# Fused gated scan, token mixing and two MLPs on one core: the opening's loads and instruction lists reordered, four value buffers, token mixing with its rows in two parts

## What is computed

```python
mag = np.sqrt(a_re * a_re + a_im * a_im)
scale = np.minimum(mag, 0.999) / (mag + 1e-06)
for t in range(S):                       # complex gated linear recurrence, one state per head
    S_re, S_im = ar * S_re - ai * S_im + kv, ar * S_im + ai * S_re   # kv = outer(k_t, v_t)
    y[:, :, t] = einsum('bhd,bhde->bhe', q[:, :, t], S_re)
x = y.transpose(0, 2, 1, 3).reshape(B, S, H * D)
h = np.maximum(x.transpose(0, 2, 1) @ w_tok1, 0.0) @ w_tok2          # token mixing, inner width 256
u = x + h.transpose(0, 2, 1)
x = u + np.maximum(u @ w_ch1, 0.0) @ w_ch2                           # first MLP, 384 -> 1536 -> 384
xn = (x - mean(x)) / sqrt(var(x) + 1e-6) * g_ln
out = x + np.maximum(xn @ w2_ch1, 0.0) @ w2_ch2                      # second MLP
```

## Time and profile before

| | |
|---|---|
| runs | 885.18, 884.48, 885.17 us |
| profiled execution | 885.37 us, of which the span of its instructions is 883.3 us |
| PE busy | 827.5 us (94%), mean granted clock 0.982 |
| DVE, ACT, GpSimd busy | 472.0 us (53%), 421.9 us (48%), 25.3 us (3%) |
| DMA | 71.15 MB, mean 81 GB/s |
| PE's first product | 24.67 us into the span |
| first `up` product of the MLP | 119.43 us into the span |

### The profile page before, as it was taken

The page is one execution under the profiler, slowest core; times in us unless marked ns, Lnnn a source line. Parts: engine busy times, 40 slices in busy tenths (PEclk is TensorE's granted clock), DMA queues, the critical chain, the costliest instruction groups (busy, mean ns, idle before and its releaser), DMA issues.

```text
span 883.3 us, 16477 instructions
## 1 busy us (share of the span) xinstructions
PE 827.5 (94%) x6890; PEld 805.5 (91%) x6890; DVE 472.0 (53%) x811; ACT 421.9 (48%) x760; POOL 25.3 (3%) x39
## 2 busy tenths in 40 slices
PE   0677899999999999999999999999999999999998
PEld 0566799999999999999999999999999999999997
DVE  7786787787586787577743644263133213312121
ACT  8866977877476777377743422222112111211111
POOL 1001001000000010001000000000000000000000
PEclk9869999999999999999999999999999999999999
DMA  9949845454434464135533500000020002000000
GB/s 374 232 66 239 200 77 123 82 109 89 101 81 83 89 134 113 45 88 105 98 64 113 182 1 1 1 1 28 1 81 1 28 1 81 27 1 27 1 27 27
DMA packets 46556, 71.15 MB, mean 81 GB/s; under 512 B 5008, under 2 KB 38032, under 8 KB 45968
## 3 DMA queue, kind: packets, MB, share of 16 engines
q1 hardware_dynamic: 46480, 70.09, 33.1%
HBM read 42.86 MB, written 8.26 MB: 58 GB/s over the span
## 4 chain that ended last, share of the span: by engine, by line
PE 49%; DMA 1%; DVE 1%; SPq 0%; issue 0%; ACT 0%; DVEq 0%
PE bank L367 16%; PE bank L369 16%; PE bank L368 16%; PE bank L1685 1%; DMA rows<-hats 1%; PE bank L1594 0%; SPq L520 0%; PE bank L1612 0%; PE bank L1616 0%; PE bank L1582 0%; DVE turned_x L1334 0%; DVE x_u L1273 0%; DVE hats L1188 0%; DVE qk_t L1175 0%; PE bank L1629 0%
## 5 line engine op out<-in xcount | busy, mean ns | idle before, releaser
L803 ACT ACTIVATE hidden<-bank 128x384 fp32r<-128x384 f32 x192 | 94.1, 490 | 347.3 <-PE bank L369 346.9
L1258 DVE SCALAR_TENSOR_TENSOR hidden<-bank,hidden 128x384 fp32r<-128x384 f32 x192 | 106.1, 553 | 256.6 <-ACT hidden L803 256.4
L369 PE MATMUL bank<-ch,hidden 128*128 128x384 f32 x576 | 192.9, 335 | 0.0
L367 PE MATMUL bank<-ch,hidden 128*128 128x384 f32 x576 | 192.7, 335 | 0.0
L368 PE MATMUL bank<-ch,hidden 128*128 128x384 f32 x576 | 192.4, 334 | 0.0
L367 PEld LDWEIGHTS bank<-ch,hidden 128*128 128x128 f32 x576 | 108.1, 188 | 0.9 <-DVE hidden L1258 0.5
L368 PEld LDWEIGHTS bank<-ch,hidden 128*128 128x128 f32 x576 | 108.1, 188 | 0.0
L369 PEld LDWEIGHTS bank<-ch,hidden 128*128 128x128 f32 x576 | 108.1, 188 | 0.0
L367 PE MATMUL bank<-turned_x,ch 128*128 128x384 f32 x288 | 102.6, 356 | 1.9 <-DVE turned_x L1334 1.9
L369 PE MATMUL bank<-turned_x,ch 128*128 128x384 f32 x288 | 96.9, 336 | 0.0
L368 PE MATMUL bank<-turned_x,ch 128*128 128x384 f32 x288 | 96.8, 336 | 0.0
(11 more groups left out here) (176 smaller groups left out, 1432.3 us busy)
## 6 DMA issues: line engine op xcount, KB each, us to landing
rows<-hats SPq DMA_DIRECT2D x120, 128.5 KB, 4.7
a_t<-in_a_rows_dram SPq DMA_DIRECT2D x18, 384.0 KB, 5.3
qk_t<-in_qk_rows_dram SPq DMA_DIRECT2D x18, 384.0 KB, 5.3
v_t<-in_v_cols_dram SPq DMA_DIRECT2D x24, 192.0 KB, 5.2
plain_ch<-in_moe_w_ch_dram SPq DMA_DIRECT2D x6, 768.0 KB, 7.2
out_dram<-x_u SPq DMA_DIRECT2D x24, 192.0 KB, 2.0
x_kept_dram<-x_u SPq DMA_DIRECT2D x18, 192.0 KB, 3.3
x_u<-x_kept_dram SPq DMA_DIRECT2D x18, 192.0 KB, 3.2
```

Source lines behind the costliest of these rows:

```text
L367: nc.tensor.matmul(ps, lhs_h, rhs_h, start=first, stop=False, skip_group_check=True)
L369: return nc.tensor.matmul(ps, lhs_l, rhs_h, start=False, stop=final, skip_group_check=True)
L803: nc.scalar.activation(hid_h[:, m % NHID, :], hid_ps[m % 2][:, 0:HALF], ACT.Relu).then_inc(hidden_rounded, 1)
L1258: nc.vector.scalar_tensor_tensor(out=hid_l[:, m % NHID, :], in0=hid_ps[m % 2][:, 0:HALF], scalar=0.0, in1=hid_h[:, m % NHID, :].bitcast(F3 ...
```

## The change

The loads on the queue stand in another order, and rows are laid in halves with other DMAs allowed between; `v_t` has four buffers in the first batch (`v_slot`), so that a load waits for tile n-4; the lists of ACT and DVE for the opening are reordered, with the logarithm and exponential steps of unit 1 and some of unit 2 ahead of the cosines of unit 0 and fewer table switches; 34 filler products instead of 26 at the start, and 4 new ones in the first token mixing. In token mixing the first products run rt by rt, the banks are laid anew, and the transposes stand between products. The slow path's buffers move to other places.

```diff
-        v_t = alloc(a_ctx, "v_t", [P, 2, C])
+        v_t = alloc(a_ctx, "v_t", [P, 4, C])
...
+        def v_slot(n):
+            return n % 4 if n < NT else n % 2
...
         def mix_ps(b):
-            return [banks[n] for n in ((0, 1, 7, 2, 3, 4) if b else (5, 6, 7, 0, 1, 4))]
-
-        turn_ps = [banks[n] for n in (5, 6, 7, 2, 3, 4)]
+            return [banks[n] for n in ((0, 1, 7, 2, 3, 4) if b else (0, 1, 4, 5, 6, 7))]
+
+        def turn_ps(b):
+            return [banks[n] for n in ((5, 6, 7, 2, 3, 4) if b else (2, 3, 4, 5, 6, 7))]
...
             def load_v(n):
...
-                if n > 1:
-                    sp.wait_ge(outputs_ready, 2 * (n - 1))
-                    sp.wait_ge(chunk_states, links(n - 1))
-                sp.dma_start(v_t[:, n % 2, :], v_cols[n]).then_inc(loaded_v[n % 2], 16)
+                before = max((i for i in range(n) if v_slot(i) == v_slot(n)), default=None)
+                if before is not None:
+                    sp.wait_ge(outputs_ready, 2 * (before + 1))
+                    sp.wait_ge(chunk_states, links(before + 1))
+                sp.dma_start(v_t[:, v_slot(n), :], v_cols[n]).then_inc(loaded_v[v_slot(n)], 16)
...
             load_a(0)
             load_a(1)
             load_qk(0)
+            load_look(0)
+            load_v(0)
+            load_a(2)
+            load_look(1)
+            load_a(3)
             load_qk(1)
-            for i in range(LOOKS):
-                load_look(i)
+            load_v(1)
             load_piece(0)
-            load_a(2)
-            load_v(0)
-            load_v(1)
+            load_look(2)
+            load_v(2)
+            load_look(3)
             load_piece(1)
-            load_a(3)
-            lay_rows(0)
-            lay_rows(1)
+            lay_rows(0, 0)
+            lay_rows(0, 1)
+            lay_rows(1, 0)
+            load_v(3)
+            lay_rows(1, 1)
+            lay_rows(2, 0)
+            lay_rows(2, 1)
+            load_a(4)
             load_qk(2)
...
@@ decay @@
+                if n == 2:
+                    act.wait_ge(looks_done, 2)
@@ rest, ACT @@
                 keep_x(0, slow)
                 round_x(0)
-                keep_khat(1, 1)
+                keep_khat(1, 0)
                 use_logs()
+                log_abs2(2)
                 inverse_mag(2)
...
@@ opening, ACT @@
             use_turns()
             angle(0)
+            angle(1)
             use_logs()
+            log_abs2(1)
+            inverse_mag(1)
+            log_re(2)
+            square_eps(1)
+            log_eps(1)
             grow_q(0)
             shrink_k(0)
+            square(2)
+            inverse_re(2)
+            grow_q(1)
+            shrink_k(1)
             use_turns()
-            angle(1)
-            decay(0)
             abs_of_turns(0)
             cosine(0)
             sine(0)
-            use_logs()
-            log_abs2(1)
-            square(2)
+            decay(0)
+            abs_of_turns(1)
+            round_piece(act, 0)
             decay(1)
...
@@ opening, DVE @@
             carry_turns(0)
+            half_turn(1)
+            offset_turns(1)
+            sum_turns(1)
+            log_step(1)
+            log_scan(1)
+            round_turns(1)
             grown_qk(0)
+            ratio0(2)
+            wrap(1)
+            carry_turns(1)
+            inverse_check(2)
             hat(0, 0)
             hat(0, 1)
             hat(1, 0)
-            half_turn(1)
             hat(1, 1)
-            offset_turns(1)
+            grown_qk(1)
+            rest_piece(dve, 0)
             least(0)
-            sum_turns(1)
+            hat(2, 0)
             abs2(2)
...
@@ mix_tokens, PE @@
                 pe.wait_ge(khat_kept, 2 * NT * (b + 1))
+                for rt in range(RT):
+                    for j in mix_order(b) if b else (NT - 1,):
+                        mix_down(b, rt, j)
                 pe.wait_ge(pieces_split, SPLIT_AT[1])
-                for j in mix_order(b) if b else (NT - 1,):
-                    for rt in range(RT):
-                        mix_down(b, rt, j)
                 if b:
                     pe.wait_ge(x2_kept, b * NT)
...
+                    pe.wait_ge(tok_hidden_split, b * RT + 1)
                     for j in range(NT):
+                        mix_up(b, 0, j)
+                    pe.wait_ge(tok_hidden_split, b * RT + 2)
+                    for j in range(NT - 1):
+                        mix_up(b, 1, j)
+                    for i in range(CT):
+                        turn_u(b, i)
+                    mix_up(b, 1, NT - 1)
+                    for i in range(CT, 2 * CT):
+                        turn_u(b, i)
+                else:
+                    for i in range(4):
+                        keep_busy()
+                    pe.wait_ge(tok_hidden_split, RT)
+                    for j in range(NT):
+                        for rt in range(RT):
+                            mix_up(b, rt, j)
+                        if j == CT:
+                            for i in range(CT):
+                                turn_u(b, i)
...
             pe.wait_ge(hats_done, 1)
-            for i in range(26):
+            for i in range(34):
                 keep_busy()
...
                         up(m)
+                        if m == 0:
+                            for i in range(CT, 2 * CT):
+                                turn_u(0, i)
+                            pe.wait_ge(u_split, 2 * CT - 1)
```

More of the change, by code:

```diff
@@ L865, in rest @@
                 log_eps(2)
-                decay(3)
+                keep_khat(1, 1)
                 keep_x(1, slow)
                 log_re(3)
+                inverse_re(3)
                 round_x(1)
@@ L880, in rest @@
                 decay(5)
+                keep_khat(3, 0)
                 keep_x(2, slow)
-                keep_khat(3, 0)
                 round_x(2)
+                angle(3)
                 use_logs()
                 log_abs2(3)
-                inverse_re(3)
                 inverse_mag(3)
@@ L919, in rest @@
                 round_x(5)
-                keep_khat(5, 1)
-                use_logs()
-                grow_q(4)
+                round_piece(act, 5)
                 round_tok_hidden(0, 0)
                 round_tok_hidden(0, 1)
+                round_turns(4)
+                use_logs()
+                log_re(5)
+                grow_q(4)
                 shrink_k(4)
-                round_piece(act, 2)
                 square(5)
-                log_re(5)
-                inverse_re(5)
-                decay(7)
-                round_piece(act, 5)
-                log_abs2(5)
-                inverse_mag(5)
-                square_eps(5)
+                round_piece(act, 3)
                 round_u(0, 0)
@@ L937, in rest @@
                 round_u(0, 2)
+                log_abs2(5)
+                use_turns()
+                abs_of_turns(4)
+                cosine(4)
                 round_u(0, 3)
                 round_u(0, 4)
+                decay(7)
+                round_u(0, 5)
+                sine(4)
+                relu_hidden(0)
+                keep_khat(6, 0)
+                use_logs()
+                inverse_re(5)
+                relu_hidden(1)
+                round_piece(act, 6)
+                inverse_mag(5)
+                square_eps(5)
+                keep_khat(6, 1)
                 log_eps(5)
+                relu_hidden(2)
                 use_turns()
-                round_turns(4)
-                keep_khat(6, 0)
-                abs_of_turns(4)
-                relu_hidden(0)
-                cosine(4)
-                keep_khat(6, 1)
-                round_u(0, 5)
-                relu_hidden(1)
-                sine(4)
-                round_piece(act, 3)
-                relu_hidden(2)
-                round_piece(act, 6)
                 angle(5)
+                keep_x(6, slow)
+                relu_hidden(3)
                 use_logs()
                 log_re(6)
-                relu_hidden(3)
                 grow_q(5)
-                keep_x(6, slow)
-                relu_hidden(4)
                 shrink_k(5)
@@ L1040, in _ @@
             sine(0)
-            use_logs()
-            log_abs2(1)
-            square(2)
+            decay(0)
+            abs_of_turns(1)
+            round_piece(act, 0)
             decay(1)
-            inverse_mag(1)
-            square_eps(1)
-            round_piece(act, 0)
-            log_eps(1)
             look(0)
+            cosine(1)
             look(1)
-            log_re(2)
-            inverse_re(2)
             look(2)
             keep_khat(0, 0)
-            grow_q(1)
-            log_abs2(2)
-            shrink_k(1)
+            sine(1)
+            decay(2)
+            decay(3)
+            angle(2)
             keep_khat(0, 1)
-            use_turns()
-            abs_of_turns(1)
-            cosine(1)
-            angle(2)
-            decay(2)
-            sine(1)
-            keep_khat(1, 0)
```

(7 more changed lines are left out.)

248 lines of the change are left out of this document (125 added, 123 removed).

## The result

| | before | after |
|---|---|---|
| runs | 884.48 to 886.26 us, median 885.17 (4 runs) | 877.46, 875.64, 876.45, 877.97 us, median 876.96 |
| profiled execution | 885.37 us, span 883.3 | 877.46 us, span 875.7 |
| PE busy, mean granted clock | 827.5 us, 0.982 | 821.8 us, 0.994 |
| first `up` product | 119.43 us | 111.44 us |

What follows compares the result with a forecast made beforehand. PE was taken as the bound after the first `up` product at 119.43 us, with idles and half-clock stretches before it. Opening -12.7 and later mixings -0.8 made -13.5 on 885.37: 871.9 us, range 866.5 to 878.5.

Steps and rivals of the forecast that it cites:

- ACT becomes the bound: Rival for the opening: waits in ACT's nearly full list delay `keep_khat` and x, 3 to 6 us more, 875 to 878; chance 0.17.
- The late start and its cover: Opening: PE starts tile 0 5.6 us later, at 43.0; 34 fillers cover the first rows, and the flag product makes it good.
- No wait for values: Tiles 2 to 5: PE's 5.1 us of waits for values go, since a load waits for the tile four back.
- the 3.0 us I charged: First mixing: one half-clock stretch, 1.2 us on fillers and `mix_down` plus 1.8 us on the up products.
- A new wait for `u_split` 5: First mixing, behind `up(0)` and three transpose groups: PE waits 1.0 us while ACT is in a table switch and unit 4's cosine.
- the exact term: Three later mixings: 1.03 us gained by rt order, 0.77 lost before `up` as `turn_u(3)` waits; net -0.26 each, -0.8 in all.
- The rival at 2.66 us: Rival: an ACT table switch costs 2.66 us, not 1.30, so fewer switches gain ACT 5.4 us more; 867.8 us, chance 0.01.
- between 3.18 and twice that; I take 3.18: ACT's branch after the flag, before `keep_x(0)`: its price among row transfers in flight, charged as 3.18 us.
- the branch stretches: Rival: the branch's 3.18 us are an instruction fetch that queues behind row transfers; up to +3.2 us, 875; chance 0.05.
- rows(4) "0.3 us" late, tiles 2 to 5 at 31.6 us: Tiles 2 to 5: four times 7.70 us plus small waits, 0.3 for rows(4) behind unit 3's ratio; 31.6 instead of 38.88 us.

Runs made afterwards that it cites:

- after, queue held: Changed kernel with the DMA queue waiting, before laying tile 2's rows, until ACT is through the branch and has kept x: 880.42 us, ratio 0.9939.
- before, with light traffic in it: Kernel before plus sixteen SBUF-to-SBUF DMAs with row-like packets, issued ahead of tile 2's rows: 887.88 us, ratio 1.0033.
- after, two value buffers: Changed kernel with two value buffers again, loads of tiles 2 to 5 queued behind the rows of their own tiles: 875.47 us, ratio 0.988.
- after, pieces late: Changed kernel with weight pieces 2 and 3 loaded behind tile 5's rows instead of ahead of tile 4's: 876.12 us, ratio 0.9892.
- after, transposes last: Changed kernel with the transposes of the three later mixings all behind the last up product: 874.68 us, ratio 0.9882.
- after, `keep_khat` ahead: Changed kernel with `keep_khat(1, 0)` ahead of ACT's branch, as in the kernel before: 880.8 us, ratio 0.9934.
- both corrections: Changed kernel with weight pieces 2 and 3 behind tile 5's rows and later mixings' transposes behind all up products, branch kept: 873.45 us, ratio 0.9857.

## Why the prediction was right and wrong

**The range.** That 876.96 us lies inside 866.5 to 878.5 is luck. The high end was set by "ACT becomes the bound" (875 to 878), which did not happen; two other things, the branch and the landing of rows(4), filled that room.

**Right.**
- The late start and its cover: fillers at 32.65 (forecast 32.5), tile 0 at 42.39 (43.0), the flag product at 46.14 (47.1). The first rows were never waited for.
- No wait for values.
- The clock: no low stretch from 33 to 81 us; one in the first mixing, behind the same 1.83 us of idle (2.3 forecast). It ran from 101.6 to 105.0 and took less than the 3.0 us I charged. From the end of tile 5 to `up(0)` I forecast 15.2 us and it was 12.7, so 2.5 us went in the kernel's favour.
- A new wait for `u_split` 5 of 0.98 us (1.0 forecast), and the 0.97 us before `turn_u(3)`, the exact term. The two weight-loading stops of a later mixing went from 1.80 to 1.46 us, -0.34 where I had -0.26; the whole later part gained 1.6 us for my 0.8, of which these stops are three times 0.34.
- Table switches: the load at 28.34 took 1.28 us and the next ACT instruction began at 29.63. The rival at 2.66 us stays dead. Ten switches had begun by the first `up` product, not nine: the last begins at 110.55, 0.9 us ahead of it.

```profile
28.34 1.28 ACT L675 ACT_TABLE_LOAD   x1
...
29.63 0.84 ACT L762 ACTIVATE plain_ch<-plain_ch 128x768 f32<-128x768 f32 x1
```

**Wrong, first: "between 3.18 and twice that; I take 3.18".** It was 6.74 us from the flag's copy (46.52) to `keep_x(0)`, a little over the upper bound. ACT's gap in each kernel, with the share of the 16 engines that the DMA queue took during it; the last column leaves out the wait for the flag, where there is one:

| kernel | share | gap, us | branch, us |
|---|---|---|---|
| after, queue held | 6% | 3.93 | 3.43 |
| before, with 18 DMAs gone before the branch | 30% | 2.92 | 2.92 |
| before | 32% | 3.18 | 3.18 |
| before, with light traffic in it | 38% | 3.08 | 3.08 |
| after, two value buffers | 84% | 6.45 | 5.95 |
| after, pieces late | 88% | 6.42 | 5.92 |
| after, transposes last | 94% | 6.72 | 6.23 |
| after, `keep_khat` ahead | 105% | 6.16 | 6.16 |
| after | 108% | 7.24 | 6.74 |
| both corrections | 111% | 7.12 | 6.63 |

The branch takes 2.9 to 3.4 us with engines that have room and 5.9 to 6.7 with full ones; nothing lies between. That is the rival "the branch stretches", to which I gave 0.05. The Trainium skill (Runtime: NRT & Kernel Launch, Instruction fetch mechanics) says that a taken branch out of the fetched window waits for a DMA fetch. The held queue agrees with it, since only the transfers were moved and 3.3 us went. That the missing time is that fetch is an inference: the profile calls it "issue", and shows the instruction queue's packets but not what ACT waited for. What I should have weighed is that my own forecast put rows(2) into flight at 45.5, right ahead of the branch, so the condition of the rival followed from my own dates.

**Wrong, second: rows(4) "0.3 us" late, tiles 2 to 5 at 31.6 us.** From `turn_k(2)` to the end of tile 5 it took 37.9 us. The term was made of DVE's order alone; the landing I never worked out for a tile whose transfers share the engines with others. An estimate from rows that stood in front of me is simple. A tile's rows are 6 x 128.5 = 771 KB, and at the 137 GB/s of the earlier trace rows that is 5.8 us of all 16 engines (a KB is 1024 bytes, a GB a thousand million). At one tile per 7.7 us they are busy three quarters of the time, and the 3.7 MB of loads that the queue issues between 38 and 64 us (v, gates, q and k, two pieces) need 8.6 us more at 433 GB/s. Asking for tile pace left the DMA engines little slack; the measured share from 33 to 81 us is 1.02, and it was 0.78 at the slower pace before. The parts of the 6.3 us: 4.0 us more of waiting for rows(4) and 3.2 us for tile 4 at the low clock (10.90 us instead of 7.70 from 80.90 to 91.80), less 0.8 since tile 5 takes only 6.9 us to its last product, and 0.1 of small waits less than I had allowed.

**The sum.** To the first `up` product, against my dates with the low stretch in them (101.6 + 3.0 = 104.6): -1.5 us until the flag is read, +3.6 for the branch, +0.2 to `mix_down(0)`, +0.8 to tile 2 (PE stood 0.98 us before `chunk_state(1)`, with no releaser in the profile), +6.3 in the tiles, -2.5 in the mixing: +6.8 before rounding, and 111.44 less 104.6 is 6.8. Less 0.1 from `up(0)` to tile 6, 0.8 more gained in the later part and 0.3 outside the span (1.76 us around it instead of 2.07), this is the 5.6 us between 871.9 and the profiled 877.46.

Whether the two failures hide each other is not settled. The medians say that each removed alone is worth at most 1.5 us and both together 6.6; the profiled spans say 2.1, 1.9 and 5.2, which is close to additive. How much is interaction and how much the spread of runs (875.64 to 877.97 for the change) stays open. What is shown is that neither alone gives the missing 5 us and both together do: 870.4 us, 1.5 below my forecast. That run is not the kernel I forecast, though: it leaves out the whole branch, the 3.18 us that I had charged for it included, and with the branch kept the pieces gave 0.8 us. "ACT becomes the bound" fell: after the branch PE never waited for `keep_khat` again.

## What to carry to other kernels

When a change packs an opening tighter, sum the bytes of every transfer over the new, shorter time at the rate that the trace shows for its kind: the DMA engines' share of before (0.78) says nothing of the share when the compute engines stop waiting. Order a queue by what the next tile needs, keep bulk weights out from in front of small latency-bound transfers, and try the place of a load before buying buffers for it. Where two limits lie close behind one another, take both out in one experiment as well; each alone can stay inside the noise.

## What the runs showed of the hardware

- The branch on ACT, counted from the flag or from ACT's last instruction, whichever came later, cost 2.9 to 3.4 us with the DMA queue at 38% of the engines or less during it (four kernels), and 5.9 to 6.7 us at 84% or more (six kernels). DVE stood 0.94 us at its own branch in the changed kernel and 1.61 us in the one before.
- In the changed kernel all engines were full at 391 GB/s in a stretch of mostly loads from HBM, and at 130 GB/s in one of rows from SBUF to SBUF:

```profile
66.00:68.00 2.00, 2.00 (x81) 1.95 (x79) 2.00 (x2) 1.83 (x5) 0.00 (x0) 1.00 1.05 391
...
74.00:76.00 2.00, 2.00 (x78) 1.95 (x77) 1.67 (x4) 2.00 (x4) 0.00 (x0) 1.00 1.14 130
```

  Tile 4's rows landed 7.9 us after their last issue began, 9.2 us in the changed kernel without the branch, and 5.1 us with the two weight pieces behind them.
- The low clock followed idles of PE of very different length (4.26 us before tile 4, 1.83 us in the mixing), while behind 2.49 us in tile 1 the granted clock stayed at 1.00. The length of one idle alone did not decide it.
